# A fused recurrent-attention and two-layer kernel: the second feed-forward stage in six groups of 512 tokens instead of eight of 384, and the first-layer weights queued ahead of group 2's decays

## What is computed

```
# r, k, v, w: (B=4, H=8, S=768, D=48);  u: (8, 48)
for t in range(S):
    cur = einsum('bhd,bhe->bhde', u * k_t, v_t)
    y_t = einsum('bhd,bhde->bhe', r_t, state + cur)
    state = w_t[..., None] * state + einsum('bhd,bhe->bhde', k_t, v_t)
x = y as (3072 tokens, 384)
h = x @ w_in                                   # 384 -> 2048
g = h if h >= 1, 0 if h <= -1, (h+1)**2/4 between
x = g @ w_out                                  # 2048 -> 384
silu = (x @ w_gate) * sigmoid(x @ w_gate)      # 384 -> 1536
out = (silu * (x @ w_val)) @ w_out2            # 1536 -> 384
```

## Time and profile before

| | before |
|---|---|
| median of 3 runs | 987.07 us (986.09 to 987.66) |
| the profiled execution's own time | 988.26 us |
| its span, first to last instruction | 986.4 us |
| TensorE (PE) busy | 961.5 us, 97% |
| VectorE (DVE) busy | 520.4 us, 53% |
| ScalarE (ACT) busy | 404.3 us, 41% |
| GpSimd (POOL) busy | 149.6 us, 15% |
| TensorE's mean granted clock | 0.996 of full speed |

### The profile page before, as it was taken

The page is one execution under the profiler, slowest core; times in us unless marked ns, Lnnn a source line. Parts: engine busy times, 40 slices in busy tenths (PEclk is TensorE's granted clock), DMA queues, the critical chain, the costliest instruction groups (busy, mean ns, idle before and its releaser), DMA issues.

```text
span 986.4 us, 17455 instructions
## 1 busy us (share of the span) xinstructions
PE 961.5 (97%) x6874; PEld 942.9 (96%) x6874; DVE 520.4 (53%) x913; ACT 404.3 (41%) x849; POOL 149.6 (15%) x146
## 2 busy tenths in 40 slices
PE   5898999999999999999999999999999999999998
PEld 4788999999999999999999999999999999999997
DVE  7795757666566675675434443434334334434332
ACT  5755546445454554554575322222222222222222
POOL 6582120210202103020253400000000000000000
PEclk9998999999999999999999999999999999999999
DMA  8816131312212122200332201010100101010000
GB/s 244 275 44 165 58 96 44 96 56 74 83 57 80 61 86 58 82 26 1 113 105 85 85 1 49 1 49 1 49 0 0 48 0 48 0 48 0 24 1 26
DMA packets 23493, 59.52 MB, mean 60 GB/s; under 512 B 2689, under 2 KB 12033, under 8 KB 23425
## 3 DMA queue, kind: packets, MB, share of 16 engines
q1 hardware_dynamic: 23424, 58.59, 18.8%
HBM read 49.14 MB, written 9.44 MB: 59 GB/s over the span
## 4 chain that ended last, share of the span: by engine, by line
PE 91%; DVE 3%; DMA 2%; issue 1%; ACT 1%; SPq 0%; POOL 0%; DVEq 0%; ACTq 0%
PE bank L1168 48%; PE bank L1196 34%; PE bank L1222 3%; PE bank L1244 2%; PE bank L1239 2%; PE bank L1250 1%; PE bank L1214 1%; PE bank L1231 1%; DMA r_k_v_by_token<-in_rkv_token 1%; DMA ring<-in_w_gate 1%; DVE glo L1019 1%; DVE gate L1026 0%; DVE suf L929 0%; DVE state_decayed L980 0%; DMA ring<-in_w_out 0%
## 5 line engine op out<-in xcount | busy, mean ns | idle before, releaser
L770 ACT ACTIVATE ghi<-gate 128x384 fp32r<-128x384 f32 x224 | 117.2, 523 | 190.6 <-DVE gate L1038 95.4
L1019 DVE TENSOR_TENSOR glo<-gate,ghi 128x384 fp32r<-128x384 f32 x224 | 133.0, 594 | 114.8 <-ACT ghi L770 112.4
L1036 DVE TENSOR_TENSOR gate<-bank,gate 128x384 f32<-128x384 f32 x96 | 53.5, 558 | 215.0 <-ACT gate L889 215.0
L1168 PE MATMUL bank<-xhi,w2gv_ahi 128*128 128x384 f32 x480 | 161.3, 336 | 0.0
L1168 PE MATMUL bank<-xlo,w2gv_ahi 128*128 128x384 f32 x480 | 161.3, 336 | 0.0
L1168 PE MATMUL bank<-xhi,w2gv_alo 128*128 128x384 f32 x480 | 161.3, 336 | 0.0
L889 ACT ACTIVATE gate<-bank 128x384 f32<-128x384 f32 x96 | 47.2, 492 | 227.7 <-PE bank L1168 227.7
L1196 PE MATMUL bank<-ghi,w1ohi 128*128 128x384 f32 x384 | 134.5, 350 | 0.7 <-DVE glo L1019 0.7
L1168 PE MATMUL bank<-xhi,w1ihi 128*128 128x384 f32 x384 | 129.5, 337 | 5.0 <-DVE gate L1026 2.3
L1196 PE MATMUL bank<-glo,w1ohi 128*128 128x384 f32 x384 | 129.7, 338 | 0.0
L1196 PE MATMUL bank<-ghi,w1olo 128*128 128x384 f32 x384 | 129.6, 337 | 0.0
(11 more groups left out here) (93 smaller groups left out, 1532.0 us busy)
## 6 DMA issues: line engine op xcount, KB each, us to landing
r_k_v_by_token<-in_rkv_token SPq DMA_DIRECT2D x24, 576.0 KB, 5.3
k_r_by_channel<-in_kr_channel SPq DMA_DIRECT2D x24, 448.0 KB, 4.1
w_by_channel<-in_w_channel SPq DMA_DIRECT2D x24, 226.2 KB, 2.7
x_t<-ring SPq DMA_DIRECT2D x8, 576.0 KB, 3.0
x_raw<-x_t SPq DMA_DIRECT2D x8, 576.0 KB, 4.0
ring<-in_w_out SPq DMA_DIRECT2D x22, 192.0 KB, 3.4
out_t<-ring SPq DMA_DIRECT2D x7, 576.0 KB, 3.1
ring<-in_w_gate SPq DMA_DIRECT2D x12, 192.0 KB, 2.3
```

The lines of the kernel that those rows point to most:

```text
L770: e.activation(ghi[j % 2][:, :], gate[j % 2][:, :], ACT.Copy).then_inc(M["hi", ph], 1)
L1019: e.tensor_tensor(glo[j % 2][:, :], gate[j % 2][:, :], ghi[j % 2][:, :].bitcast(F32), ALU.subtract)\
L1036: e.tensor_tensor(q, hid[j % 2][:, 0:T], q, ALU.mult).then_inc(M["t", 2], 1)
L1168: m = e.matmul(out, w_of(a, k), x_of(b_, k), start=start and i == 0, stop=stop and i == total - 1)
```

## The change

The second stage runs in `NG2` = 6 groups of `T2` = 512 tokens; all its matmuls, its ScalarE and VectorE operations, the `x_raw` load and the output store become 512 columns wide. Its x tiles no longer share the first stage's `xhi` and `xlo` but get places of their own: one pair behind the first weight tiles where the attention's tiles were, one pair where the first stage's output weights were, each moved on by 32 bytes, so that weights and x tiles keep their 32-byte difference by 64. To make room, `RING` goes from 13 to 11, `NA` (the j's whose gate and value weights fit over the attention) from 10 to 8, and the output weights are cut into two tiles of which the second has to wait for the last `tile_out` of the first stage. `order2` follows. The first load of `x_raw` needs two stored groups of the first stage. In SP's program, all 32 chunks of first-layer weights now stand ahead of group 2's decays.

```diff
-RING = 13
+T2 = 512
+NG2 = B * S // T2
+RING = 11
...
-        NA = 10
-        xr, o = place("x_raw", [P, KT, T], F32, att_at)
+        NA, NO = 8, 8
+        xr, o = place("x_raw", [P, KT, T2], F32, att_at)
...
+        o += 32
+        x2_a = []
+        for n in ("hi", "lo"):
+            t, o = place(f"x2{n}0", [P, KT, T2], F32R, o)
+            x2_a.append(t)
...
+        w2ob, o = [], w1o_at
+        for n in ("hi", "lo"):
+            t, o = place(f"w2o_b{n}", [P, J2 - NO, DM], F32R, o)
+            w2ob.append(t)
+        o += 32
+        x2_b = []
...
-            n = 2 + 6 * (j - NA)
-            order2 += [(j, 0), (j, 1)] + [(i, 2) for i in range(n, n + 6 if j < J2 - 1 else J2)]
+            n = 2 + 3 * (j - NA)
+            order2 += [(j, 0), (j, 1)] + [(i, 2) for i in range(n, n + 3 if j < J2 - 1 else J2)]
...
-            load_w1(14)
+            load_w1(2 * J1)
             for w in range(NW):
                 load_w(2, w)
-            load_w1(2 * J1)
...
-                e.dma_start(xr[:, :, :], half_of(x2_d, g)).then_inc(ldx, 16)
-
-            wait(M["st", 1], 32)
+                e.dma_start(xr[:, :, :], x2_d[:, :, columns(g, T2)]).then_inc(ldx, 16)
+
+            wait(M["st", 1], 48)
...
+                if s == 2 and jj == NO:
+                    e.wait_ge(M["out", 1], (NG + 1) * J1)
...
-                        m = e.matmul(acc[k][:, 0:T], wo[a][:, j, k * P:(k + 1) * P], gs[b_][:, :],
+                        m = e.matmul(acc[k][:, 0:TOK[ph]], wo(a, j)[:, k * P:(k + 1) * P], gs[b_][:, 0:TOK[ph]],
...
-                xs = (xhi[parity], xlo[parity])
+                xs = x2t[parity]
                 for s, out in ((0, hid[j % 2]), (1, attb[j % 2])):
-                    m = products(out[:, 0:T], lambda a, k: w2gv(a, j, s)[:, k * P:(k + 1) * P],
+                    m = products(out[:, :], lambda a, k: w2gv(a, j, s)[:, k * P:(k + 1) * P],
```

More of the change, by code:

```diff
@@ L125, in place @@
             return nc.alloc_sbuf_tensor_at(name, shape, dt, offset=offset), offset + size
+        x_at = at[0]
         xhi = [place(f"xhi{i}", [P, KT, T], F32R)[0] for i in range(2)]
         xlo = [place(f"xlo{i}", [P, KT, T], F32R)[0] for i in range(2)]
-        gate = [place(f"gate{i}", [P, T], F32)[0] for i in range(2)]
-        ghi = [place(f"ghi{i}", [P, T], F32R)[0] for i in range(2)]
-        glo = [place(f"glo{i}", [P, T], F32R)[0] for i in range(2)]
+        gate_at = at[0]
+        gate = [place(f"gate{i}", [P, T2], F32)[0] for i in range(2)]
+        ghi = [place(f"ghi{i}", [P, T2], F32R)[0] for i in range(2)]
+        glo = [place(f"glo{i}", [P, T2], F32R)[0] for i in range(2)]
         ring, _ = place("ring", [P, KT + RING2, T], F32)
@@ L242, in build_program @@
         J = {1: J1, 2: J2}
+        TOK = {1: T, 2: T2}
+        STAGE = {1: stage, 2: stage2}
         def state_pairs(w, parity):
@@ L297, in phase2 @@
                 slot(0, j, 0)
-            with e.Fori(0, NG // 2 - 1) as b:
+            with e.Fori(0, NG2 // 2 - 1) as b:
                 for hf in (1, 2):
@@ L302, in phase2 @@
             for j in range(J2):
-                slot(NG - 1, j, 1, True)
+                slot(NG2 - 1, j, 1, True)
         def credit(e, names, ph):
@@ L585, in half @@
                 wait(M["ed", 1], g + 2)
-                e.dma_start(half_of(x2_d, g), stage[:, :, :]).then_inc(M["st", 1], 16)
+                e.dma_start(x2_d[:, :, columns(g, T)], stage[:, :, :]).then_inc(M["st", 1], 16)
             for g in range(NG - 2):
@@ L620, in half2 @@
                 wait(M["ed", 2], g + 2)
-                e.dma_start(half_of(out_d, g), stage[:, :, :]).then_inc(M["st", 2], 16)
+                e.dma_start(half_of(out_d, g), stage2[:, :, :]).then_inc(M["st", 2], 16)
             half2(0, True)
-            with e.Fori(0, NG // 2 - 1) as b:
+            with e.Fori(0, NG2 // 2 - 1) as b:
                 for hf in (1, 2):
@@ L629, in store_k @@
             def store_k(k):
[L630 removed]
+                e.dma_start(out_d[NG2 - 1][:, k, :], stage2[:, k, :]).then_inc(M["st", 2], 16)
             wait(fin_a, 1)
@@ L637, in _ @@
             store_k(1)
-            wait(M["st", 2], 16 * NG + 3 * 16)
+            wait(M["st", 2], 16 * NG2 + 3 * 16)
             with e.If(flagged > 0):
@@ L875, in split_x @@
                 e.wait_ge(ldx, (g + 1) * 16)
[L876 to L880, removed]
+                if isinstance(g, int) and g == 1:
+                    e.wait_ge(M["out", 1], (NG + 1) * J1)
+                elif not isinstance(g, int):
                     e.wait_ge(M["h", 2], (g - 1) * J2)
-                e.activation(xhi[parity][:, :, :], xr[:, :, :], ACT.Copy).then_inc(x2hi, 1)
+                e.activation(x2t[parity][0][:, :, :], xr[:, :, :], ACT.Copy).then_inc(x2hi, 1)
             def sig(g, j):
@@ L1312, in slot @@
                         do_fill(g + 1, f, 1 - parity)
-                tile_out(1, g, j, w1o)
+                tile_out(1, g, j, lambda a, i: w1o[a][:, i, :])
             phase1(e, slot)
@@ L1326, in slot2 @@
                     e.wait_ge(M["ed", 1], NG + 1)
-                tile_out(2, g, j, w2o, last and j == J2 - 1)
+                tile_out(2, g, j, w2out, last and j == J2 - 1)
             phase2(e, slot2)
```

84 lines of the change are left out of this document (49 added, 35 removed).

## The result

The changed kernel takes **988.02 us** (median of 22 runs, 985.96 to 991.18), the kernel before 986.01 us on the same chips (22 runs, 983.47 to 989.29): ratio 1.002, 95% interval 1.0012 to 1.0029. It is 2.0 us slower; 973.6 us was predicted, with a range of 970 to 984. In the profiled executions the two spans are 986.2 and 986.4 us; the one of before lies 2.2 us above its median, so the traces show no difference where the medians show 2 us.

The account below looks back on a forecast made before the run. TensorE was taken to bound the kernel, matmul count times pace in the second stage. Terms -8.6 - 5.9 + 0.7 + 0.3 = -13.5 us gave 974.8 from the profiled 988.26, 973.6 us as median; range 970 to 984 us, 0.80.

Parts of the forecast that it names:

- Not every address relation is kept ... I price this at nothing: Second stage: new x tiles move against the weights by 256 bytes; priced at zero because all tile mixes had one pace.
- (a): Second-stage matmuls: the 13.3 ns over the columns is a fixed price per matmul, 226.7 ns at 512 columns, 8.6 us less.
- (b): Second-stage matmuls: the rest grows with the columns, 231.1 ns at 512, no gain there, 982.2 us; chance 0.08.
- (c): Second-stage matmuls: no rest at 512 columns, 213.3 ns, 34.6 us less there, 947.6 us; chance 0.10.
- Rival 3: `tile_in2`: new x tiles collide with weight reads, 13.3 ns more on 18 of 27 matmuls, 17.3 us, 991 us; chance 0.08.
- The smaller ring costs nothing by the same count: First-layer weight chunks: ScalarE wants two a slot and the ring runs five slots ahead, so 11 buffers cost zero.
- The load order: First stage, 77 to 90 us: chunks ahead of group 2's decays remove TensorE's 2.87 us wait and slow clock, -5.9 us.
- Seam and end: Between stages the larger first `x_raw` load costs +0.7 us; at the end the larger last copy and store cost +0.3 us.
- The second stage's 8.6 us: Second stage: 1944 matmuls at 226.7 ns take 440.6 us in place of 2592 at 173.3 ns, 449.3 us.

Follow-up runs that it names:

- The timed runs: Kernel before with only the changed order of loads, still 13 ring buffers and 384 columns: 981.62 us, ratio 0.9955.
- kernel alike by 256 bytes, with 13 buffers: Changed kernel with 13 ring buffers, 32-byte steps removed and second-stage hidden tiles moved, all its tiles and weights at 224 by 256: 973.45 us, ratio 0.9870.
- run with the widths: Changed kernel with each second-stage slot's gate and value matmuls at its own width, 512 down to 128 columns, leaving out columns: 904.77 us.

## Why the prediction was wrong

1. **Step that failed: "Not every address relation is kept ... I price this at nothing".** The price was 6.7 ns on each of 1,944 matmuls, 13.0 us, the whole forecast gain but 0.5 us. The reason given, that before all mixes of tiles had one pace, held only for what the kernel before has: one distance and one width. There x and hidden tiles lie 160 bytes after their weights by 256 in both stages, and at 384 columns this costs nothing over the 13.3 ns. At 512 columns the same 160 bytes cost 8.0 ns in `tile_out`, whose tiles kept their distance, and the 32 bytes of the moved x tiles cost 6.0 ns in `tile_in2`. To keep the x tiles at 160 would not have helped (233.8 to 234.4 ns in the table): what failed is less the moved address that the prediction named than the belief that a distance that is free at 384 columns is free at 512.
2. **The fixed rest, (a), was right as far as it goes.** The 13.3 ns do not grow with the columns, but at the changed kernel's addresses they are not the whole rest at 512. 226.7 ns at 512 columns is what the runs alike by 256 bytes give to the digit, and the widths from 288 to 416 have the same 13.3 ns. (b), 231.1 ns, came close to the measured 233.3, but for another reason; (c) is out.
3. **Rival 3, slower by a collision, was the right mechanism,** with a chance of 0.08 and the wrong reach: it was thought of for `tile_in2` alone at 13.3 ns; it was 6.0 ns there and 8.0 ns in `tile_out`. By its own sum (18 of 27 matmuls) the kernel would have stayed faster up to 237 ns; with all 27 the limit is 226.7 + 13.5/1.944 = 233.6 ns, and the 233.3 measured lie just below it; that the kernel is nonetheless 2 us slower comes from the terms of 4 to 6.
4. **"The smaller ring costs nothing by the same count" failed.** Chunks in a ring were counted, not the queue: the first chunk that has to wait is issued behind 3 MB of keys and tokens and lands 11 to 13 us later. With what follows it costs 1.9 us in the mean of the traces, between nothing and 3 us in single ones.
5. **The load order** was right in place and size in the trace, 5.93 us for 5.9, all five chunks out by 66.6 us (64.5 predicted), no wait in its place. The timed runs gave 4.4 us (3.1 to 5.8).
6. **Seam and end**: +0.7 and +0.3 predicted, -0.5 and -0.1 in the traces. The first chunk landed 4.86 us after its issue, not later than the 5.68 of the earlier trace rows. The prediction's own sum was also a little off: 5.68 us by 192/1,344 are 0.8 us, not 0.7.

The sum by what was measured: ring +1.9, order -4.4, seam and end -0.6, second stage +4.3 = 1.2 us; the medians say 2.0 (1.2 to 2.9). In the kernel alike by 256 bytes, with 13 buffers, about the predicted sum of 13.5 us is found, 13.1 us: 973.45 us for 973.6, ratio 0.987. The second stage's 8.6 us are there exactly; that the total agrees so well is in part luck, since the order gave 1.5 us less than predicted and seam and end did not cost the 1.0 us put down for them.

## What to carry to other kernels

A pace that is read from one layout and one width holds for these: when a change moves or widens a tile that TensorE streams, take the distance to its weights by 256 bytes into the account, and where there is room place both alike. When a ring gets smaller, look at what stands on the queue in front of the first transfer that it holds back, not at the number of buffers. And a stage without a gap can still be several per cent from its pace: compare the ns per matmul with another width.

## What the runs showed of the hardware

With 128x128 fp32r weights loaded for each matmul at the full clock, N moving columns took N/2.4 + 13.3 to 13.6 ns from 288 to 416 columns at the distance of 32 bytes (run with the widths), N/2.4 + 13.3 ns at 384 columns and 160 bytes (kernel before) and at 512 columns and 0 or 256 bytes. At 512 columns the other distances by 256 bytes added 3 ns (64) or 5 to 9 ns (all others tried), and part of this carries over to the first five matmuls behind; at 384 columns the distance of 128 added 2.2 ns. The pace is 116.8 ns at 256 columns and stops falling at 109 to 110 ns for 192 and 128. At 512 columns and a distance of 32 bytes, the number of weight columns, 32 to 128, moved the pace by 2 ns at most. Why the rest is 13.3 ns, and what in the array or the memory has the period of 256 bytes, was not found; nor was the distance of 0 tried at 384 columns in both stages.
